# Attention to experts: rows and gate logits of a tile from one product of 144 columns, with the partial logits added on VectorE

## The chip, the core and the metric

The kernel runs on one core of a Trainium2 chip. The time is device microseconds of one execution, from the first to the last instruction of the core and the short start and stop around them. Lower is better. The engines are named as the profile names them: PE is TensorE (PEld its weight loads), DVE VectorE, ACT ScalarE, POOL GpSimd, SP SyncE, which here only issues DMAs.

## What is computed

Three layers follow one another, all in float32. The core of the reference:

```
scores = q @ k.T / sqrt(64);  ret = scores * gamma[h] ** (i - j)   (i >= j, else 0);  x = ret @ v
logits = x @ w_gate;  noisy = logits + log1p(exp(x @ w_noise)) * noise
the two largest of 8 experts per row, softmax over the two
x = sum over the two of weight * (relu(x @ w1[e]) @ w2[e])
out = (h * cos(h)) @ w_out   with h = x @ w_in
```

There are 4 sequences of 576 positions, 8 heads of 64, so 2304 rows of 512 values, 8 experts with 1024 hidden values, and a last layer with 2048. The change is in the first stage alone: attention, gate logits and the routing of rows to experts.

## The kernel before

The 2304 rows are 18 tiles of 128. Attention is computed as a recurrence: a tile's own part by scores (L1607), scaled by the decay table (`scale`, L1164, VectorE), times v (L1630), and a carried part from a state of 64 x 64 per head (L1622), which each tile updates with a decayed k (`decay_k`, L1180) times v (L1638) and `carry` (L1172, VectorE) rescales. Nine tiles hold two sequences; the fifth of nine (steps 4 and 13) is mixed, its scaling takes six operations instead of two, and the ninth (tiles 8 and 17) updates no state.

The engines run in steps. In step s TensorE computes the scores of tile s, both parts of the output of tile s-1, the state update with s-1, and for tile s-2 the gate logits and the rows. The output of a tile comes out transposed (512 values by 128 rows); ScalarE copies it to `xT` (L779). From xT TensorE computes the 16 gate and noise logits (L1658: four products that accumulate into one of two banks, where the logits of a group of 3 to 4 tiles stay until they are used) and transposes xT back into rows (L1663: four transposes into bank 5). A float32 product is two instructions in the trace, a transpose is one. ScalarE copies the rows out (L789, `x_sb`), and signals `x_done`, on which the next transposes wait.

The order on each engine is the order of the code. On ScalarE a step is: softplus of a group of tiles (L755 to L763, in steps 6, 10, 14 and 17, with two loads of function tables), xT of tile s-1, the row copy of tile s-2, and in steps 4, 5, 8, 9, 13 and 16 (`SPLIT_AT`) the high part of a chunk of expert weights (w_hi, L745). On VectorE it is: scaling of tile s, carry of tile s-1, decayed k of tile s, then second choice with running totals (steps 7, 11, 15, 18), ranks to places (`place_rows`, L1141 on, steps 8, 12, 16), first choice (`first_choice`, L1110 on, steps 6, 10, 14, 17), and the low part of the weight chunk (w_lo, L1075). TensorE counts ranks (`count`, L1578 to L1583) in steps 8, 12, 16 and 18. The next scores wait for the scaling of the tile before. GpSimd multiplies q by the decay (L701) and scatters rows to the experts' slots in DRAM.

Behind step 19 follow the experts. Their first unit starts with two blocks of rows that were scattered early (transposes L1592, copies L767 and L1266), then products L1722 (first weights) and L1734 (second weights), with relu L822 on ScalarE and the low part L1274 on VectorE.

Of the kernel before, what the change touches and what calls it, by code (L numbers as in the profile page):

```python
# [23 lines left out]
P = 128  # L24
B, H, S, D = 4, 8, 576, 64
DM = H * D
C = P
# [25 lines left out]
TB = TPB * C  # L53
SIZES = (3, 5, 5, 5)
# [95 lines left out]
def build(nc, qk, kv, noise, gates_w, weights, pairs, table, out):  # L150
# [7 lines left out]
    with ExitStack() as ctx:  # L158
# [35 lines left out]
        with ExitStack() as st:  # L194
# [8 lines left out]
            wg = keep("wg", [P, KD_TILES, 2 * E], F32, st)  # L203
            used = -(-ATTN_W // 8) * 8 + 3 * 2 * DM + 3 * 2 * DM + 2 * DM + 2 * DM + DM // 2 + 3 * 2 * DM + 2 * DM + KD_TILES * 2 * E
# [11 lines left out]
            hots = keep("hots", [C, 2, NT * E], F32, st)  # L216
            before_sum = grid("before_sum", (NT + 1) * E)
# [55 lines left out]
        chain, soft_chain, soft_done = sem("chain"), sem("soft_chain"), sem("soft_done")  # L273
        picked_done, counted, ranked, pos_done = sem("picked_done"), sem("counted"), sem("ranked"), sem("pos_done")
# [45 lines left out]
        def logit_bank(k):  # L320

            return ps[7 - k % 2]
# [358 lines left out]
        def _(pool):  # L681
            nc.gpsimd.memset(zeros_sb[:, :], 0.0).then_inc(rows_zero, 1)

            def scatter_rows(t, k):
                pool.wait_ge(pos_done, group_of(t) + 1)
                pool.wait_ge(x_done, t + 1)
# [21 lines left out]
            for t in range(LATE_FROM, NT):  # L708
                if t == LATE_FROM:
                    pool.wait_ge(out_done, NT - 1)  # L710
                elif t == LATE_FROM + 1:
                    pool.wait_ge(out_done, NT)
                elif t == LATE_FROM + 2:
                    pool.wait_ge(logit_done, NT)
# [26 lines left out]
        def _(act):  # L741
# [5 lines left out]
            def softplus(k):  # L747
                lo, hi = GROUPS[k], GROUPS[k + 1]
                n = hi - lo
                act.wait_ge(logit_done, hi)  # L750
                if k == 0:
                    act.wait_ge(q_mixed_in, 16)
                above(act, picked_done, k)
                z = logit_bank(k)[0:C, 0:n * 2 * E].rearrange("c (t e) -> c t e", e=2 * E)[:, :, E:2 * E]
# [16 lines left out]
            def step(s):  # L771
# [3 lines left out]
                if 0 <= t < NT:  # L775
                    act.wait_ge(out_done, t + 1)
                    above(act, logit_done, t - 1)
# [6 lines left out]
                t = s - 2  # L784
                if t == NT - 1:
# [283 lines left out]
        def _(dve):  # L1069
# [34 lines left out]
            def first_choice(k):  # L1104
                lo, hi, n = tiles_of(k)
                both = logit_bank(k)[0:C, 0:n * 2 * E].rearrange("c (t e) -> c t e", e=2 * E)
# [23 lines left out]
            def place_rows(k):  # L1130
                lo, hi, n = tiles_of(k)
                bank = logit_bank(k)
# [33 lines left out]

            def carry(t):
# [132 lines left out]
            for j in range(FRONT[0]):  # L1300
                x_low(0, j)
            place_rows(NG - 2)
# [266 lines left out]
        def _(pe):  # L1569
            ident = tab("ident")  # L1570

            def count(k):
                lo, hi = GROUPS[k], GROUPS[k + 1]
                n, bank = hi - lo, logit_bank(k)
                pe.wait_ge(picked_done, k + 1)
                if k == 0:
# [19 lines left out]
            def step(s):  # L1596
# [51 lines left out]
                if 0 <= t < NT:  # L1648
                    k_ = group_of(t)
# [61 lines left out]
            def first1(f, part_no):  # L1711
# [4 lines left out]
                if part_no == 0:  # L1716
                    pe.wait_ge(split_done, f + 1)
                above(pe, hs_done, i - 1)
# [231 lines left out]
```

## Time and profile before

| | us |
|---|---|
| median of 3 runs | 964.93 (964.05 to 965.29) |
| the profiled execution | 967.21 |
| its span (first to last instruction) | 965.4 |
| TensorE busy in the span | 949.5 (98%) |
| VectorE busy | 557.5 (58%) |
| ScalarE busy | 474.5 (49%) |
| attention stage, first scores to first expert product | 5.6 to 99.4 |

The granted clock of TensorE is at full speed in all 40 slices of the span. The views used are: the chain of the work that ended last; busy time of each engine in chosen stretches; and the timeline, where instructions of one kind that follow one another are one row with their count, the first number is the start in us from the span's start, the second the time from the first start to the last end, and brackets at the end give the idle time ahead and what ended it.

### The profile page before, as it was taken

The numbers are of one execution on the slowest core, as the hardware profiler recorded it, in microseconds if no ns is written. First come the engines' busy times: TensorE is split into PE (matmuls) and PEld (weight loads), VectorE is DVE, ScalarE is ACT, GpSimd is POOL, SyncE is SP. The second block draws the span as 40 slices with busy tenths as digits, with TensorE's granted clock in tenths as the row PEclk, the third lists the DMA queues.
The fourth block names the chain that finished last, engine by engine and source line by source line (L and its number), as shares of the span: only waits on it lengthen the run. The fifth ranks groups of instructions, "written<-read, shape, count | busy, mean of one in ns | idle before, by whom it ended". The sixth has DMA issues, their size and how long they took to land.

```text
span 965.4 us, 17039 instructions
## 1 busy us (share of the span) xinstructions
PE 949.5 (98%) x6144; PEld 846.1 (88%) x6144; DVE 557.5 (58%) x1118; ACT 474.5 (49%) x889; POOL 95.0 (10%) x93
## 2 busy tenths in 40 slices
PE   8999899999999999999999999999999999999998
PEld 7988788988989889889898889888888888888987
DVE  4789554455555545534332145567777777776665
ACT  1445434434434344333232156567666765766555
POOL 2266600000000000000000123001100100000000
PEclk9999999999999999999999999999999999999999
DMA  9988546598879897874317259877666755656561
GB/s 363 325 329 284 197 161 231 175 299 307 294 281 316 292 329 249 261 253 135 122 65 270 68 169 326 279 277 259 241 256 226 263 216 234 237 205 238 218 236 55
DMA packets 77406, 230.29 MB, mean 239 GB/s; under 512 B 6781, under 2 KB 31005, under 8 KB 69149
## 3 DMA queue, kind: packets, MB, share of 16 engines
q1 hardware_dynamic: 71581, 210.58, 61.7%
q0 software_dynamic: 5760, 18.88, 5.4%
q8 instruction: 37, 0.61, 0.2%
q14 instruction: 28, 0.23, 0.1%
HBM read 167.75 MB, written 61.69 MB: 238 GB/s over the span
## 4 chain that ended last, share of the span: by engine, by line
PE 82%; DVE 7%; ACT 6%; issue 3%; DMA 2%; POOL 0%; SPq 0%; DVEq 0%
PE ps L1704 18%; PE ps L1686 17%; PE ps L1879 14%; PE ps L1865 11%; PE ps L1734 3%; PE ps L1722 3%; PE ps L1805 3%; PE ps L1793 2%; PE ps L1630 2%; PE ps L1607 2%; PE ps L1622 2%; ACT angle L968 2%; PE ps L1658 2%; PE ps L1592 2%; ACT angle L966 1%
## 5 line engine op out<-in xcount | busy, mean ns | idle before, releaser
L1879 PE MATMUL ps<-w_sb,g_hi 128*128 128x512 f32 x576 | 180.4, 394 | 0.1
L1686 PE MATMUL ps<-xs,w_hi 128*128 (+1 forms) x784 | 177.7, 308 | 0.0
L1287 DVE TENSOR_TENSOR w_lo<-raw,w_hi 128x1024 fp32r<-128x1024 f32 x48 | 58.8, 1225 | 157.2 <-ACT w_hi L807 157.2
L1686 PEld LDWEIGHTS ps<-xs,w_hi 128*128 128x128 f32 x784 | 131.7, 188 | 1.2
L1865 PE MATMUL ps<-x_odd,w_sb 128*128 128x320 f32 x672 | 117.7, 310 | 2.1 <-DVE h_sb L1442 1.2
L1686 PE MATMUL ps<-xs,w_lo 128*128 (+1 forms) x392 | 119.1, 304 | 0.0
L1865 PEld LDWEIGHTS ps<-x_odd,w_sb 128*128 128x128 f32 x672 | 106.2, 188 | 14.5 <-DVE h_sb L1442 2.5
L807 ACT ACTIVATE w_hi<-raw 128x1024 fp32r<-128x1024 f32 x48 | 50.8, 1058 | 129.6 <-PE ps L1704 126.1
L1879 PE MATMUL ps<-w_sb,g_lo 128*128 128x512 f32 x288 | 112.5, 391 | 0.0
L1879 PEld LDWEIGHTS ps<-w_sb,g_hi 128*128 128x128 f32 x576 | 101.0, 188 | 9.8 <-issue 0.3
L1704 PE MATMUL ps<-w_hi,hs_lo 128*128 128x512 f32 (+1 forms) x245 | 97.0, 396 | 0.0
L1704 PE MATMUL ps<-w_lo,hs_hi 128*128 128x512 f32 (+1 forms) x245 | 96.3, 393 | 0.0
L727 POOL DMA_INDIRECT y<-y_slots,pos_i x36 | 35.4, 982 | 615.5 <-SPq L647 429.2
L1704 PE MATMUL ps<-w_hi,hs_hi 128*128 128x512 f32 (+1 forms) x245 | 95.4, 389 | 0.0
L801 ACT ACTIVATE hs_hi<-ps 128x308 fp32r<-128x308 f32 x98 | 41.6, 424 | 68.0 <-PE ps L1686 68.0
L974 ACT ACTIVATE g_hi<-angle 128x320 fp32r<-128x320 f32 (+1 forms) x112 | 53.7, 479 | 43.2 <-DVE angle L1457 38.0
L966 ACT ACTIVATE angle<-angle 128x320 f32<-128x320 f32 (+1 forms) x112 | 53.5, 478 | 42.9 <-DVE angle L1451 41.3
L1686 PEld LDWEIGHTS ps<-xs,w_lo 128*128 128x128 f32 x392 | 73.7, 188 | 0.9
L1462 DVE TENSOR_TENSOR g_lo<-angle,g_hi 128x320 fp32r<-128x320 f32 (+1 forms) x112 | 56.1, 501 | 30.8 <-ACT g_hi L974 20.8
L1457 DVE TENSOR_TENSOR angle<-h_sb,angle 128x320 f32<-128x320 f32 x96 | 47.2, 491 | 45.5 <-ACT angle L968 43.7
L960 ACT ACTIVATE turns<-h_sb 128x320 f32<-128x320 f32 x96 | 44.9, 468 | 44.7 <-DVE h_sb L1440 41.6
L968 ACT ACTIVATE angle<-angle,table_sb 128x320 f32<-128x320 f32 (+1 forms) x112 | 64.0, 571 | 3.6
(193 smaller groups left out, 1606.2 us busy)
## 6 DMA issues: line engine op xcount, KB each, us to landing
w_sb<-w_pairs SPq DMA_DIRECT2D x24, 1792.0 KB, 7.7
w_sb<-w_pairs SPq DMA_DIRECT2D x40, 1024.0 KB, 10.0
raw<-weights SPq DMA_DIRECT2D x64, 512.0 KB
w_pairs<-stage SPq DMA_DIRECT2D x24, 1024.0 KB, 7.1
qk<-qk SPq DMA_DIRECT2D x18, 512.0 KB
kv<-kv SPq DMA_DIRECT2D x18, 512.0 KB
y_slots<-zeros_sb SPq DMA_DIRECT2D x33, 256.0 KB
gath<-x_slots SPq DMA_DIRECT2D x32, 256.0 KB, 6.5
```

The lines of the kernel that those rows point to most:

```text
L807: nc.scalar.activation(w_hi[:, f * CHUNK:(f + 1) * CHUNK], raw[:, f % 2, :], ACT.Copy).then_inc(hi_done, 1)
L960: nc.scalar.activation(turns[c % 2][:, 0:n], h[:, 0:n], ACT.Copy, bias=ROUND).then_inc(turn_done, 1)
L966: nc.scalar.activation(a, a, ACT.Abs).then_inc(abs_done, 1)
L968: nc.scalar.activation(a, a, ACT.Sin, scale=-2.0 * np.pi, bias=tab("half_pi")).then_inc(sin_done, 1)
L974: nc.scalar.activation(g_part(g_hi, slot, q), angle[c % 4][:, 0:width(slot)], ACT.Copy).then_inc(g_hi_done, 1)
L1287: tt(w_lo[:, at], raw[:, f % 2, :], w_hi[:, at].bitcast(F32), ALU.subtract).then_inc(split_done, 1)
L1457: tt(angle[c % 4][:, 0:n], h_of(slot, q)[:, 0:n], angle[c % 4][:, 0:n], ALU.mult).then_inc(g_done, 1)
L1462: tt(g_part(g_lo, slot, q), angle[c % 4][:, 0:n], g_part(g_hi, slot, q).bitcast(F32), ALU.subtract).then_inc(g_split, 1)
L1686: last_one = nc.tensor.matmul(ps[5 + half][:, 0:HALF], w[:, at:at + P], xs[:, bass.ds(g % 2, 1), a, k, half * HALF:(half + 1) * HALF].rear ...
L1704: last_one = nc.tensor.matmul(ps[j][0:ROWS[j], :], a[:, f % 2, rows_of(j)], w[:, at:at + DM], start=f == 0 and i == 0, stop=f == FE - 1 an ...
L1865: last_one = nc.tensor.matmul(p_bank(i)[:, 0:n], w[:, hl, cols], x[:, a, m, k, :], start=k == 0 and j == 0, stop=k == 1 and j == 2)
L1879: last_one = nc.tensor.matmul(ps[j][:, :], a[:, slot % 2, part, j * C:(j + 1) * C], w2_sb[slot % 3][:, hl, part * DM:(part + 1) * DM], sta ...
```

## The change

The gate weights in SBUF get 144 columns for each of the four parts of a row instead of 16: the 16 columns of weights and the 128 columns of a unit matrix, in this order or the other by turns. One product of such a part with xT gives the transposed rows and a partial sum of the logits. Two parts share a bank (5 and 6): they are laid so that the 16 logit columns of both fall on the same columns and accumulate. So each bank holds 256 row values and half of the logits. VectorE adds the halves into SBUF (`sum_logits`, new, two operations of 128 x 16), in step s for tile s-3, behind the scaling. TensorE's product waits for both row copies and for the sum of the tile before, and all readers of the logits read SBUF. The wait of the first tile of a group for earlier ranks is gone; rank counts all use bank 7. The row copy is two instructions of 256 columns. The last tile keeps four logit products (bank 4) and four transposes (bank 3), and the second chunk of the first expert product waits for its row copy. The sums of tiles 16 and 17 are made behind the experts' first `x_low`. In the last step the row copy stands ahead of the last softplus.

```diff
@@ ACT, step @@
                 t = s - 2
+                if 0 <= t < NT:
+                    act.wait_ge(rows_ps_done, t + 1)
+                    for k in range(0, KD_TILES, 2):
+                        rows = row_bank(k)[0:C, 0:2 * GW].rearrange("c (k d) -> c k d", d=GW)[:, :, 0:P]
...
+                        nc.scalar.activation(x_sb[t][:, k * P:(k + 2) * P].rearrange("c (k d) -> c k d", d=P), rows,
+                                             ACT.Copy).then_inc(x_done, 1)
                 if t == NT - 1:
                     softplus(NG - 1)
-                if 0 <= t < NT:
-                    act.wait_ge(rows_ps_done, t + 1)
-                    nc.scalar.activation(x_sb[t][:, :], ps[5][0:C, :], ACT.Copy).then_inc(x_done, 1)
@@ DVE @@
+            def sum_logits(t):
+                if t == NT - 1:
+                    dve.wait_ge(rows_ps_done, NT)
+                else:
+                    dve.wait_ge(x_done, 2 * t + 2)
+                logits = both_sb[:, t * 2 * E:(t + 1) * 2 * E]
+                if t == NT - 1:
+                    nc.vector.tensor_copy(logits, LAST_LOGITS[0:C, 0:2 * E]).then_inc(logit_done, 1)
+                else:
+                    nc.vector.tensor_copy(logits, row_bank(0)[0:C, P:P + 2 * E]).then_inc(half_done, 1)
+                    dve.wait_ge(half_done, t + 1)
+                    tt(logits, row_bank(2)[0:C, P:P + 2 * E], logits, ALU.add).then_inc(logit_done, 1)
...
             for s in range(NT + 1):
                 if s < NT:
                     scale(s)
+                if 0 <= s - 3 < NT - 2:
+                    sum_logits(s - 3)
                 if 0 < s <= NT and (s - 1) % CB < CB - 1:
                     carry(s - 1)
...
                 x_low(0, j)
+            for t in range(NT - 2, NT):
+                sum_logits(t)
             place_rows(NG - 2)
@@ PE, step @@
-                    if t == GROUPS[k_]:
-                        above(pe, ranked, k_ - 1)
                     pe.wait_ge(xT_done, t + 1)
-                    at = (t - GROUPS[k_]) * 2 * E
-                    for k in range(KD_TILES):
-                        last_one = nc.tensor.matmul(logit_bank(k_)[0:C, at:at + 2 * E], xT[t % 2][:, k, :], wg[:, k, :],
-                                                    start=k == 0, stop=k == KD_TILES - 1)
-                    last_one.then_inc(logit_done, 1)
-                    above(pe, x_done, t)
+                    if t == NT - 1:
+                        pe.wait_ge(state_done, updates(t))
...
+                        return
+                    above(pe, x_done, 2 * t)
+                    above(pe, logit_done, t)
                     for k in range(KD_TILES):
-                        last_one = nc.tensor.transpose(ps[5][0:C, k * P:(k + 1) * P], xT[t % 2][:, k, :], ident)
+                        at = P * (k % 2)
+                        last_one = nc.tensor.matmul(row_bank(k)[0:C, at:at + GW], xT[t % 2][:, k, :], wg[:, k, :],
+                                                    start=k % 2 == 0, stop=True, skip_group_check=True)
                     last_one.then_inc(rows_ps_done, 1)
```

How the work stands on VectorE around step 5 before the change (line, operation, output<-inputs, shape, and the semaphores waited for): the low part of a weight chunk, the scaling of tile 5, carry, decayed k.

```order
L1172 TENSOR_TENSOR state<-ps,attn_table 128x256 [waits u_done]
L1180 TENSOR_TENSOR k_dec<-kv,attn_table 128x512 [waits u_done,kv_in1]
L1075 TENSOR_TENSOR w_lo<-raw,w_hi 128x1024 [waits hi_done]
L1164 TENSOR_TENSOR ret<-ps,attn_table 128x512 [waits scores_done] x2
L1172 TENSOR_TENSOR state<-ps,attn_table 128x256 [waits u_done]
L1180 TENSOR_TENSOR k_dec<-kv,attn_table 128x512 [waits u_done,kv_in2]
```

The same place in the changed kernel, whose line numbers differ (L1177 is the scaling, L1198 carry):

```order
L1198 TENSOR_TENSOR state<-ps,attn_table 128x256 [waits u_done]
L1206 TENSOR_TENSOR k_dec<-kv,attn_table 128x512 [waits u_done,kv_in1]
L1088 TENSOR_TENSOR w_lo<-raw,w_hi 128x1024 [waits hi_done]
L1177 TENSOR_TENSOR ret<-ps,attn_table 128x512 [waits scores_done] x2
L1189 COPY both_sb<-ps 128x16 [waits x_done]
L1191 TENSOR_TENSOR both_sb<-ps,both_sb 128x16 [waits half_done]
L1198 TENSOR_TENSOR state<-ps,attn_table 128x256 [waits u_done]
L1206 TENSOR_TENSOR k_dec<-kv,attn_table 128x512 [waits u_done,kv_in2]
```

Two short operations stand between the scaling and carry; nothing else moved. On TensorE, the end of a step before:

```order
L1638 MATMUL ps<-kv,k_dec 64x64 [waits k_dec_done]
L1638 MATMUL ps<-kv,k_dec 64x64 x7
L1658 MATMUL ps<-wg,xT 128x16 [waits xT_done]
L1658 MATMUL ps<-wg,xT 128x16 x3
L1663 MATMUL ps<-table_sb,xT 128x128 [waits x_done]
L1663 MATMUL ps<-table_sb,xT 128x128 x3
L1607 MATMUL ps<-qk 128x128 [waits ret_done,qk_in0]
```

And in the changed kernel:

```order
L1669 MATMUL ps<-kv,k_dec 64x64 [waits k_dec_done]
L1669 MATMUL ps<-kv,k_dec 64x64 x7
L1698 MATMUL ps<-wg,xT 128x144 [waits logit_done,x_done,xT_done]
L1698 MATMUL ps<-wg,xT 128x144 x3
L1638 MATMUL ps<-qk 128x128 [waits ret_done,mixed_done,qk_in2]
```

Eight products and transposes became four products, and the first of them waits for the sum (`logit_done`) and the row copies (`x_done`) of the tile before.

## Rows read from the trace of the kernel before

**Rows 1.** The chain of work that ended last, shares of the span by engine.

```profile
PE 82%; DVE 7%; ACT 6%; issue 3%; DMA 2%; POOL 0%; SPq 0%; DVEq 0%
```

**Rows 2.** Busy time in stretches: steps 5, 9 and 10 of attention.

```profile
core 0: us, PE busy (x) PEld busy (x) DVE busy (x) ACT busy (x) POOL busy (x), PEclk, DMA share, GB/s
...
27.10:32.16 5.06, 5.06 (x78) 4.53 (x78) 3.47 (x6) 2.14 (x3) 1.27 (x1) 1.00 1.00 347
...
47.85:52.47 4.62, 4.62 (x62) 3.99 (x62) 3.17 (x5) 2.14 (x3) 2.77 (x3) 1.00 0.71 280
52.47:56.65 4.18, 4.06 (x61) 3.66 (x61) 2.44 (x4) 4.07 (x7) 3.70 (x4) 1.00 0.95 329
```

**Rows 3.** The chain in step 5: start us, us, engine, output, line, instructions.

```profile
27.09 1.09 PE ps L1607 x16
28.18 1.02 PE ps L1622 x16
29.20 1.02 PE ps L1630 x16
30.22 0.46 PE ps L1638 x16
30.68 0.99 PE ps L1658 x8
31.68 0.48 PE ps L1663 x4
```

**Rows 4.** Timeline of steps 4 and 5 (start us, us, engine, line, operation).

```profile
26.45 0.64 PE L1663 MATMUL ps<-table_sb,xT 128*128 128x128 f32 x4
...
27.12 0.60 ACT L789 ACTIVATE x_sb<-ps 128x512 f32<-128x512 f32 x1 [1.34 <-PE ps L1663]
27.61 1.05 ACT L745 ACTIVATE w_hi<-raw 128x1024 fp32r<-128x1024 f32 x1
...
28.70 1.22 DVE L1075 TENSOR_TENSOR w_lo<-raw,w_hi 128x1024 fp32r<-128x1024 f32 x1 [1.58 <-ACT w_hi L745]
...
29.84 1.28 DVE L1164 TENSOR_TENSOR ret<-ps,attn_table 128x512 f32<-128x512 f32 x2
```

**Rows 5.** Timeline of ScalarE and VectorE: softplus, first choice, scaling, steps 6 and 7.

```profile
33.64 0.19 ACT L755 ACTIVATE soft_a<-ps 128x32 f32<-128x32 f32 x1
...
35.40 0.32 ACT L760 ACTIVATE soft_a<-soft_b,attn_table 128x32 f32<-128x32 f32 x1
...
37.15 0.58 ACT L779 ACTIVATE xT<-ps 128x512 f32<-128x512 f32 x1
...
37.20 0.18 DVE L1110 SCALAR_TENSOR_TENSOR t_c<-ps,soft_a 128x32 f32<-128x32 f32 x1
37.41 0.19 DVE L1111 TENSOR_TENSOR t_b<-t_c,noise_sb 128x32 f32<-128x32 f32 x1
...
38.75 0.19 DVE L1101 TENSOR_TENSOR hots<-t_b,code 128x32 f32<-128x32 f32 x1
38.98 1.29 DVE L1164 TENSOR_TENSOR ret<-ps,attn_table 128x512 f32<-128x512 f32 x2
```

**Rows 6.** Timeline of ScalarE: two copies of 256 columns out of PSUM.

```profile
102.53 0.65 ACT L822 ACTIVATE hs_hi<-ps 128x256 fp32r<-128x256 f32 x2
```

**Rows 7.** Timeline of step 4, the mixed tile: scores, scaling's first and last operation.

```profile
21.93 1.16 PE L1607 MATMUL ps<-qk 64*128 64x128 f32 x16
...
23.20 0.27 DVE L1160 MEMSET ret<- 64x256 f32 x1 [1.18 <-PE ps L1607]
...
25.34 0.69 DVE L1164 TENSOR_TENSOR ret<-ps,attn_table 64x512 f32<-64x512 f32 x1
```

**Rows 8.** Timeline of TensorE at the stage's end, steps 17 to 19.

```profile
91.84 1.06 PE L1658 MATMUL ps<-wg,xT 128*128 128x16 f32 x8
...
96.30 0.96 PE L1658 MATMUL ps<-wg,xT 128*128 128x16 f32 x8
...
97.58 0.30 PE L1578 MATMUL ps<-picked,attn_table 128*128 128x24 f32 x2
...
99.43 0.36 PE L1722 MATMUL ps<-xs,w_hi 128*128 128x256 f32 x1
```

More of the change, by code:

```diff
@@ L53 @@
 TB = TPB * C
+GW = P + 2 * E
 SIZES = (3, 5, 5, 5)
@@ L202, in build @@
             xT = [keep(f"xT{i}", [P, KD_TILES, C], F32, st) for i in range(2)]
-            wg = keep("wg", [P, KD_TILES, 2 * E], F32, st)
-            used = -(-ATTN_W // 8) * 8 + 3 * 2 * DM + 3 * 2 * DM + 2 * DM + 2 * DM + DM // 2 + 3 * 2 * DM + 2 * DM + KD_TILES * 2 * E
+            wg = keep("wg", [P, KD_TILES, GW], F32, st)
+            used = -(-ATTN_W // 8) * 8 + 3 * 2 * DM + 3 * 2 * DM + 2 * DM + 2 * DM + DM // 2 + 3 * 2 * DM + 2 * DM + KD_TILES * GW
             keep("below_rows", [P, 2 * RING * CHUNK + TPU * DM - used], F32, st)
@@ L216, in build @@
             hots = keep("hots", [C, 2, NT * E], F32, st)
+            both_sb = keep("both_sb", [C, NT * 2 * E], F32, st)
             before_sum = grid("before_sum", (NT + 1) * E)
@@ L318, in group_of, with row_bank, logits_of @@
             return next(k for k in range(NG) if GROUPS[k] <= t < GROUPS[k + 1])
-        def logit_bank(k):
-            return ps[7 - k % 2]
+        def row_bank(k):
+            return ps[5 + k // 2]
+        def logits_of(t, n):
+            return both_sb[:, t * 2 * E:(t + n) * 2 * E].rearrange("c (t e) -> c t e", e=2 * E)
+        COUNTS, LAST_LOGITS, LAST_ROWS = ps[7], ps[4], ps[3]
         def x2_bank(n):
@@ L784, in step @@
                 t = s - 2
+                if 0 <= t < NT:
[3 more added lines that the diff above has]
+                        if t == NT - 1:
+                            rows = LAST_ROWS[0:C, k * P:(k + 2) * P].rearrange("c (k d) -> c k d", d=P)
+                        nc.scalar.activation(x_sb[t][:, k * P:(k + 2) * P].rearrange("c (k d) -> c k d", d=P), rows,
+                                             ACT.Copy).then_inc(x_done, 1)
                 if t == NT - 1:
                     softplus(NG - 1)
-                if 0 <= t < NT:
-                    act.wait_ge(rows_ps_done, t + 1)
-                    nc.scalar.activation(x_sb[t][:, :], ps[5][0:C, :], ACT.Copy).then_inc(x_done, 1)
                 if s in SPLIT_AT:
@@ L1105, in first_choice @@
                 lo, hi, n = tiles_of(k)
-                both = logit_bank(k)[0:C, 0:n * 2 * E].rearrange("c (t e) -> c t e", e=2 * E)
+                both = logits_of(lo, n)
                 if k == 0:
@@ L1131, in place_rows @@
                 lo, hi, n = tiles_of(k)
-                bank = logit_bank(k)
+                bank = COUNTS
                 dve.wait_ge(counted, k + 1)
@@ L1573, in count @@
                 lo, hi = GROUPS[k], GROUPS[k + 1]
-                n, bank = hi - lo, logit_bank(k)
+                n, bank = hi - lo, COUNTS
                 pe.wait_ge(picked_done, k + 1)
+                above(pe, ranked, k)
                 if k == 0:
@@ L1652, in step @@
                         pe.wait_ge(wg_in, 16)
-                    if t == GROUPS[k_]:
-                        above(pe, ranked, k_ - 1)
                     pe.wait_ge(xT_done, t + 1)
-                    at = (t - GROUPS[k_]) * 2 * E
-                    for k in range(KD_TILES):
-                        last_one = nc.tensor.matmul(logit_bank(k_)[0:C, at:at + 2 * E], xT[t % 2][:, k, :], wg[:, k, :],
-                                                    start=k == 0, stop=k == KD_TILES - 1)
-                    last_one.then_inc(logit_done, 1)
-                    above(pe, x_done, t)
-                    for k in range(KD_TILES):
-                        last_one = nc.tensor.transpose(ps[5][0:C, k * P:(k + 1) * P], xT[t % 2][:, k, :], ident)
+                    if t == NT - 1:
+                        pe.wait_ge(state_done, updates(t))
+                        for k in range(KD_TILES):
+                            at = P * (1 - k % 2)
+                            nc.tensor.matmul(LAST_LOGITS[0:C, 0:2 * E], xT[t % 2][:, k, :], wg[:, k, at:at + 2 * E],
+                                             start=k == 0, stop=k == KD_TILES - 1)
+                        for k in range(KD_TILES):
+                            last_one = nc.tensor.transpose(LAST_ROWS[0:C, k * P:(k + 1) * P], xT[t % 2][:, k, :], ident)
+                        last_one.then_inc(rows_ps_done, 1)
+                        return
+                    above(pe, x_done, 2 * t)
+                    above(pe, logit_done, t)
+                    for k in range(KD_TILES):
+                        at = P * (k % 2)
+                        last_one = nc.tensor.matmul(row_bank(k)[0:C, at:at + GW], xT[t % 2][:, k, :], wg[:, k, :],
+                                                    start=k % 2 == 0, stop=True, skip_group_check=True)
                     last_one.then_inc(rows_ps_done, 1)
@@ L1717, in first1 @@
                     pe.wait_ge(split_done, f + 1)
+                    if f == 1:
+                        pe.wait_ge(x_done, 2 * NT)
                 above(pe, hs_done, i - 1)
@@ L1932 @@
     rows = moe2_w_out.reshape(FP, 2, P, DM).transpose(0, 2, 1, 3).reshape(FP, P, 2 * DM)
-    gates = np.concatenate([moe_w_gate, moe_w_noise], axis=1).reshape(KD_TILES, P, 2 * E).transpose(1, 0, 2)
+    gates = np.concatenate([moe_w_gate, moe_w_noise], axis=1).reshape(KD_TILES, P, 2 * E)
+    unit = np.eye(P, dtype=np.float32)
+    gates = np.stack([np.concatenate([unit, g] if k % 2 == 0 else [g, unit], axis=1) for k, g in enumerate(gates)], axis=1)
     arrays = {
```

9 lines of the change are left out of this document (4 added, 5 removed).

## The prediction

> **What bounds the kernel now.** I read the chain of work that ended last first: 82% of its span is TensorE [rows 1]. Then the busy time by stretch, over steps of the attention stage: TensorE is busy for all of a step's 5.06 us and for all of the 4.62 us of step 9 [rows 2]. So the 18 tiles cost what TensorE's own instructions cost, and the stage is worth shortening. The chain of one step, step 5 [rows 3], gives the parts: scores 1.09 us, carried part 1.02, own part 1.02, state update 0.46, the four logit products 0.99, the four row transposes 0.48. That is 5.06 us, and the logits are reached 3.59 us after the scores begin (30.68 against 27.09).
>
> Then the timeline of the same step, for the slack of the others [rows 4]. VectorE scales the scores of step 5 only from 29.84, though they are ready at about 28.2: ahead of the scaling stands w_lo (28.70), which waits for w_hi (27.61), which stands on ScalarE behind the copy of the rows (27.12), which waits for the transposes of the step before, ended at 27.09. The scaling ends at 31.12. Today nothing needs it before the next scores at 32.16, so a lateness of one microsecond costs nothing. This is the cover that the change uses up.
>
> **What it removes.** Four transposes (0.48 us) and four 16-column products (0.99) become four products of 144 columns, eight instructions instead of twelve. A 16-column piece takes 0.99/8 = 124 ns, so it is paced by loading 128 weight columns and not by its columns. How long 144 columns take no row shows. Below: 0.99 us, if the load still paces them. Above: pairs of half-array products take 0.46/8 = 58 ns at 64 columns and 1.02/8 = 128 ns at 128 [rows 3], 1.09 ns for each column more, which makes 145 ns at 144 and 1.16 us for eight. I take the middle, 1.07: 0.40 us less a tile, and 17 tiles give 6.8 us. The last tile keeps its 1.47.
>
> The Trainium skill speaks against this trade: Perfetto Trace Analysis, section Transposes, says that a logical transpose should be a transpose and not a standard matmul, since transposes skip the arithmetic. By that rule the unit columns would cost a pass of their own and the product would save nothing, 1.47 us. The rows speak against the rule here, since the weight load is paid by the logits anyway; it is a rival below.
>
> **What it adds.** On VectorE, right behind each scaling, two [128 x 16] operations that sum the logits of the tile three back. The product of step s now waits for that sum, since both banks are used again. The nearest operations take 0.18 us, follow one another in 0.21 where the second waits for the first (37.20, 37.41) and overlap the next by 0.08 where it doesn't (28.70 + 1.22 against 29.84) [rows 4, 5]. So a sum ends 0.30 us behind the scaling, TensorE restarts 0.10 later, and VectorE loses 0.31 a step; bounds 0.20 (nothing waited for) and 0.42 (both in full). On the dependence between the two: the Trainium skill, VectorE: DVE Perf Modes, section The DRAIN you can't avoid, says that an operation starts only when the pipe is empty, semaphore or not. That would make it 0.42 and the forecast 1.3 us later; w_lo and the scaling overlap by 0.08 us here, so the trace doesn't agree.
>
> The row copy in two halves costs 0.65 against 0.60 us [rows 4, 6]. The weights of the gates grow from 32 to 288 KB; at the rate of the first stretches that is under a microsecond of a queue whose next users have more slack, and I cost it at nothing; without the cover it is 0.7 us.
>
> **What becomes late.** TensorE's own step would be 5.07 - 0.40 = 4.67 us. Three kinds of steps can't be that short.
>
> Steps 5, 6, 9, 10, 14 and 17, whose scaling stands behind w_lo. From the end of the transposes to the end of the scaling it is 31.12 - 27.09 = 4.03 us; the second copy adds 0.05, the sum and the restart 0.40, the product and its end 1.17. This closes a circle (product, row copy, w_hi, w_lo, scaling, sum, product) of 5.65 us. Four of these steps take 5.07 now: 4 x 0.58 = 2.3. Steps 9 and 10 lack a part of TensorE's work and take 4.62 and 4.18 [rows 2], so they lose 1.03 and 1.47. Together 4.8 us.
>
> Steps 7, 11 and 15, behind a first choice. Softplus now waits for the sum behind the scaling: 2.08 us of ScalarE (33.64 to 35.72), 1.78 of first choice (37.20 to 38.98), 1.29 of scaling [rows 5], 0.30 of sum and 0.1 of handovers make 5.55 from product to product. 3 x 0.48 = 1.4 us.
>
> Steps 4 and 13, where the tile has two sequences: its scaling goes from 23.20 to 26.03, which is 4.10 us after the scores began at 21.93 [rows 7]. With 0.40 the product starts at 4.50 instead of 3.59: 0.9 less the 0.40 saved is 0.5. In step 13 VectorE comes from placing ranks and is later still, I take 0.8. Together 1.3 us.
>
> Steps 2, 3, 8, 12 and 16 wait for nothing and keep the gain, 5 x 0.40 = 2.0 us.
>
> The stage up to step 18: 4.8 + 1.4 + 1.3 - 2.0 = 5.5 us later. Then step 18: the sum of tile 15 waits for its row copy, and that copy stands on ScalarE behind softplus, table loads and xT. From the sum of tile 14: 3.51 us (33.64 to 37.15), 0.49, 0.65 and 0.4 make about 5.1 between the two products, now 4.46 (91.84 to 96.30) [rows 5, 8]: 0.6. Behind that sum stands the second choice with its totals, 2.24 us, and the rank count waits for it: 2.3 us after the product, now 1.28 (96.30 to 97.58): 1.0. The last tile (logits 0.99, transposes 0.48) and the first expert product behind it (now 99.43) follow as now, and I see nothing that gives time back: the experts' first half starts with data that was long loaded, and its late rows are scattered on a count of TensorE's own products. Sum: 5.5 + 0.6 + 1.0 = 7.1, say 7.0 us. The profiled execution takes 967.21 us (span 965.4 and 1.8 around it) and would take 974.2; from the median 964.93 it is 971.9.
>
> Bounds: product 0.99 and sum 0.20 take 1.3 and 1.3 us off (16 steps, 12 waits), product 1.16 and sum 0.42 add 1.4 and 1.3: 969.3 to 974.6.
>
> **Rivals.** (a) The waits don't come and the gain stays: 964.93 - 6.8 = 958.1, faster. One mechanism: VectorE reaches the sum before TensorE reaches the product. For this the scaling would have to end 0.4 us before product time, 3.59 us into a step; in step 5 it ends at 4.03, in step 4 at 4.10. The point from which it decides is 0.9 us of lateness; what speaks for it are only the five steps in which VectorE is in time. (b) The circles hold loosely, waits of half the size: +1 to +4 us, about 967.4. For it: steps are coupled, and a late TensorE lets VectorE catch up. Against it: each circle contains the product itself, so lateness doesn't cure it. (c) The unit columns cost a pass, product 1.47, which lengthens the twelve late steps by 0.40 each: +4.8, 976.7. (d) Waits and gain cancel, within 0.2%: seven waits instead of twelve.
>
> **Chances.** Forecast (969.3 to 974.6) 0.72, (a) 0.10, (b) 0.08, (c) 0.05, (d) 0.05. 0.2% is 1.9 us, about what a measurement of this kernel can tell from no change: faster 0.10, same 0.05, slower 0.85. The range reaches to (b) and (c), 966.5 to 976.8, and leaves (a) and most of (d) out.
>
> **What would show it.** After: eight 144-column pieces in 1.0 to 1.16 us; TensorE idle ahead of the product, released by the sum, twelve times with 0.9 to 2 us, some 13 us in all; steps of 5.65 us where w_lo stands ahead and of 4.67 in steps 3, 8 and 16; VectorE's scaling and sum back to back; first expert product at about 106.5 instead of 99.43, and the same length behind it. It is wrong if TensorE's idle time ahead of the product is under 5 us, if the product takes over 1.3 us, or if the experts' part changes by more than a microsecond.

## The result and the profile after

The changed kernel takes 980.29 us (median of 4 runs, 978.89 to 982.29) against 964.71 beside it: ratio 1.0153, 95% interval 1.0137 to 1.0168. It is slower, and by more than forecast: 971.9 with a range up to 976.8. The profiled execution has a span of 977.6 us (979.43 in all) against 965.4. The traces so show 12.2 us of difference, where the medians show 15.6; the profiled execution of the kernel before lies 2.5 us above its median, that of the changed one 0.9 below. What follows is about the 12.2; the other 3.4 no trace shows.

What TensorE waited for in the changed kernel, in all three layers (engine, output and line, releaser: us in total, times, longest). L1698 is the product of 144 columns, L1191 the sum, L1623 the transposes of late rows, L1818 the transposes in the last layer.

```profile
PE ps L1698 <- DVE both_sb L1191: 12.5, 12, 2.0
PE ps L1623 <- DMA gath<-x_slots: 3.7, 3, 3.0
PE ps L1818 <- DVE y L1411: 2.1, 1, 2.1
```

Twelve waits, 12.5 us, from 0.7 to 2.0 us each. The prediction said twelve, 0.9 to 2 us, some 13 in all, and they stand in the twelve steps that it named. The chain that ended last, cut to step 5 (start us, us, engine, output, line, instructions), answers to [rows 3], which was TensorE alone from start to end:

```profile
26.24 1.23 PE ps L1698 x8
27.47 0.02 issue
27.50 0.03 ACT x_sb L799
27.52 0.25 issue
27.77 0.38 ACT x_sb L799
28.15 0.96 ACT w_hi L754
29.11 0.02 issue
29.13 1.23 DVE w_lo L1088
30.36 1.20 DVE ret L1177 x2
31.55 0.09 DVE both_sb L1189
31.65 0.02 issue
31.67 0.18 DVE both_sb L1191
31.86 0.14 issue
31.99 1.23 PE ps L1698 x8
```

This is the circle, link by link: product, row copy, high part, low part, scaling, sum, product again, 31.99 - 26.24 = 5.75 us. The same stretch in the timeline (brackets: idle time ahead, and what ended it), which answers to [rows 4]:

```profile
28.04 1.06 ACT L754 ACTIVATE w_hi<-raw 128x1024 fp32r<-128x1024 f32 x1
...
29.13 1.23 DVE L1088 TENSOR_TENSOR w_lo<-raw,w_hi 128x1024 fp32r<-128x1024 f32 x1 [2.11 <-ACT w_hi L754]
...
30.27 1.28 DVE L1177 TENSOR_TENSOR ret<-ps,attn_table 128x512 f32<-128x512 f32 x2
...
31.99 1.22 PE L1698 MATMUL ps<-wg,xT 128*128 128x144 f32 x8 [0.93 <-DVE both_sb L1191]
```

VectorE's 2.11 us of idle time ahead of w_lo are the heart of it. VectorE is idle for want of ScalarE's high part, and the scaling and the sum that TensorE needs stand behind.

The lengths of the steps, from the first scores of one to those of the next:

| step | 2 | 3 | 4 | 5 | 6 | 7 | 8 | 9 | 10 | 11 | 12 | 13 | 14 | 15 | 16 |
|---|---|---|---|---|---|---|---|---|---|---|---|---|---|---|---|
| before | 5.07 | 5.08 | 5.08 | 5.08 | 5.08 | 5.08 | 5.53 | 4.62 | 4.25 | 5.08 | 5.75 | 5.07 | 5.08 | 5.08 | 5.53 |
| after | 4.77 | 4.78 | 5.81 | 5.75 | 5.75 | 5.64 | 5.22 | 5.75 | 5.75 | 5.56 | 5.45 | 6.04 | 5.75 | 5.56 | 5.23 |

The end of the stage on TensorE, which answers to [rows 8]. L1653 is the carried part, L1609 the rank count, L1688 and L1691 logits and transposes of the last tile, L1760 the first expert product, L1772 the first one with second weights:

```profile
99.44 1.22 PE L1698 MATMUL ps<-wg,xT 128*128 128x144 f32 x8 [0.93 <-DVE both_sb L1191]
100.59 1.09 PE L1653 MATMUL ps<-q_dec,state 64*64 64x128 f32 x16
...
104.61 1.22 PE L1698 MATMUL ps<-wg,xT 128*128 128x144 f32 x8 [0.88 <-DVE both_sb L1191]
106.51 0.40 PE L1609 MATMUL ps<-picked,attn_table 128*128 128x24 f32 x2 [0.68 <-DVE before_sum L1137]
...
106.97 1.54 PE L1688 MATMUL ps<-wg,xT 128*128 128x16 f32 x8
108.35 1.09 PE L1691 MATMUL ps<-table_sb,xT 128*128 128x128 f32 x4
109.10 0.56 PE L1760 MATMUL ps<-xs,w_hi 128*128 128x256 f32 x1
...
114.29 0.40 PE L1772 MATMUL ps<-w_hi,hs_hi 128*128 128x512 f32 x1
```

The last tile's logits, whose instructions are those of before, take 1.38 us from start to start (106.97 to 108.35) instead of 1.08 in the same place before (97.94 to 99.02), and its transposes 0.75 (to 109.10) instead of 0.41 (to 99.43). The reason stands in the busy time by stretch (stretch, PE busy, PEld, DVE, ACT, POOL, then the granted clock):

```profile
104.61:106.90 2.29, 1.61 (x12) 1.40 (x12) 2.01 (x10) 1.49 (x4) 0.60 (x1) 1.00 0.55 213
106.90:114.20 7.30, 7.30 (x39) 7.30 (x39) 4.17 (x20) 2.88 (x7) 3.53 (x4) 0.53 0.24 94
114.20:118.00 3.80, 3.80 (x24) 3.41 (x24) 2.62 (x14) 1.07 (x3) 0.75 (x2) 1.00 0.25 96
```

For 7.3 us TensorE runs at a granted clock of 0.53, about the lower of its two levels (1.2 instead of 2.4 GHz), while it is busy all the time. In the eight us before 106.5 it had waited 0.93, 0.88 and 0.68 us. In the kernel before the clock is full in this place.

So the difference grows along the trace: +7.3 us at the carried part of tile 17 (100.59 against 93.32), +8.3 at the last wide product (104.61 against 96.30), +8.9 at the rank count, +9.7 at the first expert product, +10.9 at the first second-weights product (114.29 against 103.42), +11.3 at the experts' second part, +11.1 at the start of the last layer, +12.2 at the end, the last step of it behind the one wait of 2.1 us at L1818 above.

### The profile page after: what moved, and what is told of

Read it like the earlier page. It is cut to its first block, busy times and chain, and to the rows that moved or that the text cites. A ratio compares the mean times of both kernels' runs of the same rounds, so it can differ in the third digit from the quotient of the medians.

```text
span 977.6 us, 16976 instructions
## 1 busy us (share of the span) xinstructions
PE 947.7 (97%) x6076; PEld 844.3 (86%) x6076; DVE 559.9 (57%) x1153; ACT 476.2 (49%) x907; POOL 95.2 (10%) x93
## 4 chain that ended last, share of the span: by engine, by line
PE 72%; DVE 10%; ACT 8%; issue 5%; DMA 3%; POOL 1%; SPq 0%; DVEq 0%; POOLq 0%
PE ps L1740 17%; PE ps L1722 17%; PE ps L1917 13%; PE ps L1903 11%; PE ps L1831 2%; PE ps L1843 2%; PE ps L1772 2%; ACT angle L981 2%; PE ps L1623 2%; PE ps L1760 2%; DVE angle L1487 2%; ACT angle L979 2%; DVE ret L1177 1%; PE ps L1698 1%; DVE angle L1481 1%
```

## The experiments

All ratios are to the kernel before, run on the same chip in turns. Line numbers in rows of an experiment are its own.

**1. The wait without the product.** The kernel before, its products and transposes as they were, with two dummy operations on VectorE where the sum would stand, and TensorE's logit product waiting for them:

```diff
                 if s < NT:
                     scale(s)
+                if 0 <= s - 3 < NT - 2:
+                    extra(s - 3)        # copy and add, 128 x 16, on its own memory
@@ PE @@
+                    if t < NT - 1:
+                        above(pe, extra_done, t)
```

> The kernel before, with the wait alone: two small VectorE operations on spare data (128 x 16, the second waits for the first) behind each scaling from step 3 on, and TensorE's logit products of step s wait for them as the wide product does in the changed kernel. Products, transposes, banks and row copies stay as before. Theory (the wait behind the scaling is the whole cost): TensorE waits some 11 us in twelve steps, the first expert product starts at 111 to 113 us, time 978 to 986. Rival (the wide product, its banks and the halved row copies are what costs): within 2 us of the kernel before, 964.7.

Measured: 985.24 us, ratio 1.0197 (1.0182 to 1.0212). Its first expert product starts at 119.74 us, 20.3 later than before and some 7 later than expected. Steps 13, 14 and 16 take 6.81, 6.47 and 6.47 us (scores at 82.34, 89.15, 95.62, then 100.69 and 107.16) where they took 5.07, 5.08 and 5.53; step 16 does not even wait in the changed kernel. The clock is full in these steps, so this is the wait itself.

It is not so in the whole stage. The rows show TensorE's waits for the two operations, then the stretch from the scores of step 2 to the first expert product, with the same instructions but for one, here and in the kernel before:

```profile
PE ps L1670 <- DVE extra_sb L1172: 10.4, 8, 2.2
12.16:119.74 107.58, 97.19 (x1267) 87.06 (x1267) 76.35 (x212) 40.37 (x67) 41.80 (x37) 0.90 0.76 267
11.78:99.43 87.65, 87.50 (x1266) 78.63 (x1267) 68.91 (x177) 39.55 (x66) 43.72 (x37) 1.00 0.91 326
```

Of the 19.9 us that the stretch is longer, some 10.2 are waiting and 9.7 are the same work at a lower granted clock: 0.90 in the mean, 0.50 in 60 to 66 us, behind a wait of 2.2 us. So the added wait, with the clock that falls when it comes, is enough to lose more than the change loses. The waits alone are not: they are 10.4 us, where the changed kernel has 12.5.

**2. The same work, waited for by nobody.** The same two operations, without the two lines on PE.

> The kernel before with two more operations of 128 x 16 on VectorE behind each scaling, the second waiting for the first, as the changed kernel has them, but on memory of their own, and no other engine waits for them. The same two operations with TensorE's logit product waiting for them gave 985.2 us against 965.8. Theory (the wait costs, not the work): 0.3 us of VectorE a step move the scaling of steps 5 and others a little, but the next scores had a microsecond of slack; 965.5 to 968. Rival (VectorE is so full that its load alone sets the steps, the wait only shows it): 16 x 0.31 us come through in most of the late steps, 970 or more.

Measured: 968.60 against 968.40, ratio 1.0009 (1.0000 to 1.0018). Its first expert product is 2.0 us late (101.42), and at the end of the span 1.3 of that are left against the trace of before (966.7 and 965.4). So of the 2% of experiment 1 about 1.9 come with the wait, half of it as waiting and half as a lower clock: VectorE is 58% busy in the span and has time for the work; it does not have it at the moment at which TensorE asks.

This trace holds something else: the clock falls behind the rank count here too, though TensorE had waited 0.27 us in the ten before 101.2. A stretch just behind the first expert product:

```profile
102.00:103.00 1.00, 1.00 (x6) 1.00 (x6) 0.29 (x2) 0.98 (x2) 0.88 (x1) 0.50 0.21 82
```

So a fall of the clock needs no long wait just ahead of it.

**3. The sum ahead of the scaling.** The changed kernel, with the sum of the tile three back ahead of the scaling of this step:

```diff
             for s in range(NT + 1):
+                if 0 <= s - 3 < NT - 2:
+                    sum_logits(s - 3)
                 if s < NT:
                     scale(s)
-                if 0 <= s - 3 < NT - 2:
-                    sum_logits(s - 3)
```

> The changed kernel, with one edit: VectorE sums the logits of tile s-3 ahead of the scaling of tile s instead of behind it. Nothing else moves. Theory (the circles through the scaling make the changed kernel slow): the row copies of tile s-3 are done by then, so VectorE doesn't wait, TensorE's idle time ahead of the wide product falls from about 13 us in all to under 4, steps come down from 5.75 to 4.8 us, and the first expert product starts at about 97 us against 109.1 in the changed kernel and 99.4 in the one before. With few waits the clock stays at full level. Time 961 to 963.5 us. Rival (the wide product of 1.17 us and VectorE's added work cost what was lost, wherever the sum stands): it stays above 975.

Measured: 967.77, ratio 1.0029 (1.0013 to 1.0044). Of the 1.53% over the kernel before 1.24 are gone, some 12 us, with two instructions moved by one place. The waits for the sum fall from 12.5 us to

```profile
PE ps L1698 <- DVE both_sb L1191: 2.2, 4, 0.9
```

and steps 5, 6, 9 and 10 from 5.75 us each to 4.78, 4.78, 4.61 and 4.71. The mixed tiles come down to 4.77 and 5.03 (steps 4 and 13), two of the three steps behind a first choice to 5.02 and 4.78 (7 and 15); step 11 stays at 5.80, and no run tells why. But the expected 961 to 963.5 did not come. The first expert product starts at 98.53, 0.9 us ahead of the kernel before and not the 2.4 of the expectation: step 18 stayed long. And what was gained there was spent behind it: TensorE reaches the late rows earlier and waits 2.2 us for their DMA at 123.68, the clock is 0.50 in 126 to 130, and the last layer has a wait of 2.1 us at L1818.

**4. The high part first.** The changed kernel with the other link of the circle opened: on ScalarE the high part of the weight chunk ahead of the row copy, the sum where the change has it.

```diff
                 t = s - 2
+                if s in SPLIT_AT:
+                    split_high(SPLIT_AT[s], w_hi, SPLIT_AT[s] * CHUNK)
                 if 0 <= t < NT:
                     act.wait_ge(rows_ps_done, t + 1)
...
-                if s in SPLIT_AT:
-                    split_high(SPLIT_AT[s], w_hi, SPLIT_AT[s] * CHUNK)
```

> The changed kernel, with one edit on ScalarE: in the six steps that split a weight chunk, w_hi stands ahead of the row copy of tile s-2 instead of behind it. Theory (in steps 5, 6, 9, 10, 14 and 17 the circle product, row copy, w_hi, w_lo, scaling, sum, product of 5.75 us sets the time): the circle is cut, those six steps lose 0.6 to 1.9 us each, about 7 us together, while the steps behind a first choice and the mixed ones keep their waits. First expert product at about 102, time 971 to 974. Rival (VectorE is simply out of time in these steps, in whatever order): no change from 980.3.

Measured: 974.43, ratio 1.0097 (1.0083 to 1.0112), just above the expected 971 to 974; the first expert product starts at 102.49. Steps 5, 6, 9 and 10 take 4.78, 4.78, 4.46 and 4.71 us; the mixed tiles (5.80 and 6.05) and step 11 (5.80) are as late as in the changed kernel, since high parts have nothing to do with them. The clock is 0.74 in 98 to 104 us. The waits for the sum are 4.7 us in six.

```profile
PE ps L1698 <- DVE both_sb L1191: 4.7, 6, 1.2
```

Experiments 3 and 4 open the same circle at two different links and both times the 5.75-us steps are gone. That is what shows the circle, and rules out the product and a general lack of time on an engine.

**5. The clock.** The changed kernel, with seven products of zeros in step 18, whose results nobody reads: four ahead of the last wide product, three ahead of the rank count, where TensorE had waited anyway.

```diff
                     above(pe, logit_done, t)
+                    if t == NT - 2:
+                        fill(4)
...
                 if t == NT - 2:
+                    fill(3)
                     count(NG - 2)
```

> The changed kernel, with dummy products of zeros into the spare bank 7 in step 18: four ahead of the last wide product and three ahead of the rank count, where TensorE waited 0.9 and 0.7 us. They should fit into the waits. Theory (the granted clock fell to 0.53 from 106.9 to 114.2 because TensorE had waited just before, and 3.4 us of the loss are this clock): the clock stays at full level there, the first unit's products take 119 ns instead of 213, and the time is 2.5 to 3.5 us less, about 977. Rival (the fall has nothing to do with these two waits, but with the ones before them or with something else): the clock falls all the same, 980.

Measured: 975.92, ratio 1.0114 (1.0099 to 1.0128), 4.4 us less than the changed kernel by the medians, 3.8 by the ratios. Products that compute nothing make the kernel faster. The mean granted clock of its four executions is 0.996 to 0.998, that of the changed kernel's four 0.991 to 0.995. Its stretch that answers to 106.90 to 114.20 above, with clock 1.00:

```profile
106.90:114.20 7.30, 6.71 (x50) 6.24 (x51) 5.08 (x22) 3.19 (x8) 3.84 (x4) 1.00 0.29 108
```

The rank count is even 0.3 us later than without (106.84), but the first expert product comes at 108.59 instead of 109.10 and the first second-weights product at 112.31 instead of 114.29.

By the traces the kernel is 4.9 us faster (spans 972.7 and 977.6). 2.0 of them are there at the second-weights product, 1.1 more at the experts' second part (138.66 against 141.73), behind a shorter wait for the late rows (2.2 against 3.0 us). Another 2.0 come in the last layer, where this trace lacks the wait of 2.1 us; nothing shows that the fill did that.

**6. Both moves.** Experiments 3 and 4 in one kernel.

> The changed kernel with both moves at once: the sum of the tile three back stands on VectorE ahead of the scaling, and the high part of a weight chunk stands on ScalarE ahead of the row copy. Each alone took part of the circle apart: with the sum first 2.2 us of waiting on it were left, with the high part first 4.7. Theory (the loss is the order of the queues, and two handovers make it): the waits on the sum in steps 5 to 17 go to under 1 us in all, the carried product of tile 17 starts at about 88.6 us of the span (before 93.3, sum first alone about 91.2), the first expert product at about 97 (before 99.43, sum first alone 98.53). Behind it the stall for the late rows stays, since their scatters are paced by the experts' own products and TensorE only reaches it earlier. So the time is 964 to 967 us by the stall and the halved clock behind it, 963 if the gain of the stage is kept. Rival (the stage is held by something else, VectorE's own load): the first expert product stays at 98.5 and the time at 967.8.

Measured: 967.01 against 968.40, ratio 0.9987 (0.9976 to 0.9998). The stage is now clearly shorter than before (steps 5, 6, 9, 10 at 4.78, 4.78, 4.32, 3.82), but the first expert product comes at 98.16, not at 97. TensorE still waits in step 18, and the clock falls once more behind it (0.80 in 98 to 104):

```profile
93.91 1.22 PE L1698 MATMUL ps<-wg,xT 128*128 128x144 f32 x8 [0.51 <-DVE both_sb L1191]
95.86 0.40 PE L1609 MATMUL ps<-picked,attn_table 128*128 128x24 f32 x2 [0.73 <-issue]
```

**7. Both moves, and a fill for the late rows.** Seven products of zeros ahead of the transposes of the first late rows.

```diff
+            fill(7)
             for j in range(FRONT[0], TPU):
                 transpose_x(0, j)
```

> The kernel with both moves, and seven more float32 products of 128 columns of zeros (14 instructions, some 1.85 us by the 0.26 us that one took in the filled step 18) into the bank of the rank counts, ahead of the transposes of the first late block of rows, where TensorE waited 2.2 us with the sum first. Their results are read by nobody. Theory (a halved clock follows a wait of TensorE, and the products only use time in which it waits anyway): the granted clock stays full behind the stall, where the kernel with the sum first had 0.69 in 122 to 126 us and 0.50 in 126 to 130, which cost it some 3 us; the time is 2 to 3.5 us below the kernel with both moves alone and ends at 961 to 963.5, below the kernel before. Rival (the halved clock is a matter of the moment or of the DMA traffic, not of the wait): the clock falls all the same and the time is that of the kernel without the fill, or up to 1 us above it.

Measured: 967.19, ratio 0.9994 (0.9981 to 1.0007), the same as without. The clock is full from 104 us on, where experiment 6 had 0.71 in 122 to 126, and the second part starts at 128.37 instead of 129.11. That does not bear out the theory: the fill runs from 123.70, and experiment 6 lost its clock before that, behind a wait of 2.5 us at 119.54 that the profile calls "issue" and that is 1.0 us here. The expected 2 to 3.5 us were a misreading: in experiment 6 the long stall was no longer at the late rows, so there was nothing to fill there. And this execution had one wait of 2.77 us for the sum, in the attention stage at 60.05, where experiment 6 had 0.95; it is not explained.

**8. The table load out of step 18's chain.** With both moves, ScalarE still does in step 17: softplus, a load of the next function table (1.28 us), the output copy of tile 16, the row copy of tile 15. The load moves behind the two copies.

```diff
-                if k < NG - 1:
+                if k < NG - 2:
                     nc.scalar.activation(sin_ready[:, :], tab("half_pi"), ACT.Exp)
@@ behind the row copy @@
+                if s == NT - 1:
+                    nc.scalar.activation(sin_ready[:, :], tab("half_pi"), ACT.Exp)
```

> The kernel with the sum and the high part first, and in step 17 the load of the exponential's table (1.28 us of ScalarE) stands behind the output copy of tile 16 and the row copy of tile 15 instead of ahead of them. With both moves alone these copies started at 92.16 and 92.63 us though their data was there from 88.3 and 90.0, the sum of tile 15 waited for them until 93.38, TensorE's last wide product waited 0.51 us for that sum and the rank count behind it 0.73 us, and the granted clock was 0.88 in 94 to 98 and 0.80 in 98 to 104. Theory (step 18 is a chain softplus, table, copies, sum, second choice, count): the wide product no longer waits, the count comes 0.5 to 0.9 us earlier, the first expert product at 97.0 to 97.6 instead of 98.16; 1 us off the time, ratio to before 0.9965 to 0.998. Rival (the first choice on VectorE, which ends at 92.4, holds step 18 just as well, or the time is lost again at the late rows): the first expert product within 0.3 us of 98.16, ratio 0.9985 or more.

Measured: 965.44 against 967.75, ratio 0.9980 (0.9966 to 0.9994). The wide product no longer waits, the rank count waits 0.55, and the clock stays full in 94 to 104 us (it is 0.58 in 118 to 122, behind a wait of 2.4 us). The first expert product starts at 96.19, earlier than expected:

```profile
92.74 1.15 PE L1700 MATMUL ps<-wg,xT 128*128 128x144 f32 x8
94.44 0.40 PE L1611 MATMUL ps<-picked,attn_table 128*128 128x24 f32 x2 [0.55 <-issue]
...
96.19 0.36 PE L1762 MATMUL ps<-xs,w_hi 128*128 128x256 f32 x1
```

**9. And a fill ahead of the count.** The same with `fill(3)` ahead of `count(NG - 2)`.

> The same kernel, and three products of zeros (0.83 us for three in the filled step 18) between the last wide product and the rank count, where TensorE waited 0.73 us for the second choice. Theory (it is the wait just ahead that halves the clock of the experts' first products): the granted clock is full in 96 to 104, where both moves alone had 0.80 to 0.88 (some 1.3 us lost there), the experts' first pieces follow each other in 119 ns from the start, and the second part (columns of 360) starts 1 to 1.5 us earlier than with the table load alone; ratio to before 0.995 to 0.997. Rival (what is gained ahead of the late rows is lost waiting for them): the clock is full, and the time is that of the kernel with the table load alone.

Measured: 965.10 against 967.75, ratio 0.9975 (0.9963 to 0.9988): the best kernel of the study, faster than the kernel before by 0.25%; it can't be told from experiment 8. The time is where the rival put it. The clock is full in 94 to 104:

```profile
94.00:104.00 10.00, 9.31 (x70) 8.56 (x69) 7.34 (x35) 5.56 (x15) 5.95 (x7) 1.00 0.53 210
```

but it was full without the fill too, so the fill had nothing to save here. The experts' second part starts at 125.04 us, 2.3 ahead of experiment 8 and not the expected 1 to 1.5; this trace lacks that one's wait of 2.4 us and the lower clock behind it, and nothing shows that the fill is the reason. That is 5.4 us ahead of the kernel before, and at the end of the span 1.8 are left. Most of it goes at one row:

```profile
PE ps L1826 <- DVE y L1413: 3.6, 1, 3.6
```

In the last layer TensorE waits 3.6 us for rows that are gathered from DRAM. ScalarE, which is ahead of VectorE on the same rows, had waited for the DMA itself:

```profile
578.73 0.72 ACT L899 ACTIVATE y<-y,gate 128x512 f32<-128x512 f32 x1 [3.88 <-DMA y<-y_slots,pos_i]
```

Behind TensorE's wait the granted clock is 0.81 in 581.2 to 590 us. The kernel before and experiments 1, 2 and 5 have no such wait, experiments 3, 4 and 8 and the changed kernel do (2.1, 2.0, 3.3 and 2.1 us), experiments 6 and 7 a shorter one (0.9 and 0.6). In that stretch the gathers share the DMA engines with loads of 1 MB of weights. Which order of the two makes the wait was not tried and stays open.

## Why the prediction was right in kind and wrong in size

**The direction and the mechanism held.** The three kinds of late steps are the ones that were named, and each is late by about what its circle asks for. Experiments 3 and 4 show the circle through w_lo; for the other two kinds it is the size, and that moving the sum shortens them but for step 11, that speaks for the circle. By kind, forecast and measured against the kernel before (the circle steps are 5, 6, 9, 10, 14 and 17, the last by 94.84 to 100.59 against 88.24 to 93.32; step 10 of before is 4.25 us from scores to scores, not the 4.18 of the prediction's window):

| steps | forecast | measured |
|---|---|---|
| circle through w_lo (6) | +4.8 | +5.3 |
| behind a first choice: 7, 11, 15 | +1.4 | +1.5 |
| mixed tiles: 4, 13 | +1.3 | +1.7 |
| no wait: 2, 3, 8, 12, 16 | -2.0 | -1.5 |
| start, steps 0 and 1 | 0 | +0.3 |
| up to the carried part of tile 17 | +5.5 | +7.3 |

**The product was mis-sized.** "I take the middle, 1.07." It took the upper bound. The one that waits for nothing in step 18 of experiment 8 takes 1.15 in the timeline; from the start of a waited product to the next instruction it is 31.99 to 33.14, also 1.15. In steps without a wait it is 1.18 (20.40 to 21.58), and the saving was 0.30 (5.07 to 4.77) instead of 0.40. The line drawn through two other shapes, 58 ns at 64 columns and 128 at 128 [rows 3], gave 1.16; the middle between it and "the load still paces them" had no row on its side. At 0.08 to 0.10 in each of 16 steps that is 1.3 to 1.6 of the 1.8 us missing in the stage; the rest is in the mixed tiles and the first two steps. In these the wait for the first queries and keys (L1638) is 0.9 us where it was 0.8; it is 1.1 in experiment 1 too, whose gate weights are those of before, so it does not speak for the larger weights. The circle came out 5.75 against 5.65 for it.

The rule of the Trainium skill weighed in the prediction (Perfetto Trace Analysis, section Transposes) was not borne out here: the unit columns cost no pass of their own, 1.15 to 1.18 us for the wide product against 1.47 for products and transposes apart.

**The sum was sized right.** 0.30 behind the scaling: the scaling's end is at 31.55 and the sum's at 31.85 (31.67 + 0.18). The 0.10 to TensorE's restart is 0.14. What the prediction says there against the Trainium skill (VectorE: DVE Perf Modes, section The DRAIN you can't avoid) leaves out half of it: the same section says that an operation which is not held back starts earlier, so the overlap of 0.08 us here is no evidence against it.

**Step 18 held, but the sum counted 0.4 twice.** The forecast's 0.6 is from product to product, and there it measured 0.7 (99.44 to 104.61, 5.17 against 4.46). But the 5.5 us ahead of it end where the carried part of tile 17 begins, so the product's saving in step 17 was taken off once more. From the carried part on, the prediction's own terms give 5.1 - 1.07 = 4.0 against 2.98 now, +1.0, and +1.0 was measured (4.02). So its own terms sum to 7.5 and not 7.1. From the last wide product to the rank count it was +0.6 (forecast 1.0): the count came 1.90 us behind the product and not 2.3. The two errors cancel, which is luck.

**"I see nothing that gives time back", and nothing that takes any: this step failed.** Behind the rank count the forecast was a difference that stays at 7.1, and behind the first expert product "the same length"; the cost of a lower clock stood in the sum at nothing, without a reason. The difference grew from 8.9 to 12.2, 2.5 of it behind the first expert product, where the prediction had called more than a microsecond a sign of being wrong. Of these 3.3 us, 1.9 are the clock between rank count and second weights (0.7 up to the first expert product, 1.2 up to the first product with second weights). Experiment 5 shows it: with TensorE kept busy in its waits, the same stretch runs at full clock, and the second weights start 2.0 us earlier. The section on the profile before says "at full speed in all 40 slices", and the prediction took the clock for granted. A 9 in that row of the page only means 90% or more. The trace of before had a warning in it that I did not use: behind its one long stall of TensorE in the experts' first part, the granted clock is 0.77 between 118.5 and 126 us; a slice of the page is 24 us wide and hides that. Another 1.1 us come in the last layer with its wait of 2.1. The last 0.3 is spread.

**The rivals.** (a) and (d) did not come. (b) was wrong in saying that lateness lets VectorE catch up; the waits were all there. (c) was wrong in mechanism, but its 976.7 was nearer to the time than the forecast, for a reason that it did not contain. The range ended 3.5 us below the result. Against the forecast of 7.0 us the trace is 5.2 over: 1.8 in the stage, nothing in step 18 by cancelling errors, 3.3 behind it, and rounding. The medians are another 3.4 over, and no trace says where.

## What to carry to other kernels

When an instruction is put behind another on an in-order engine and a third engine waits for it, walk the whole way round: from the waiting product back to the product before. If the way closes, its length is the length of the step, no matter how idle each engine is. The remedy is the order in the queue; here it cost nothing (0.3 us of work ahead of the scaling instead of behind it: some 12 us).

Price a TensorE that starts to wait often at more than its waits: experiment 1 had 10.4 us of waits and lost another 9.7 to a lower clock. Look at the granted clock of short stretches, not of the page's slices, behind each place where it waits already.

A gain in a stage that is followed by a chain with its own pace (here scatters, gathers, weight loads) has to be followed to the end of the span: 5.4 us of lead at the experts' second part were worth 1.8 at the end.

## What was not expected of the hardware

The granted clock fell to 0.53 after three waits of 0.7 to 0.9 us within eight, not after a long one, and stayed there for 7.3 us of unbroken work. With waits of 0.51 and 0.73 us in the same place (experiment 6) it was 0.80 in 98 to 104 us, with 0.28 and 0.68 (experiment 3) or one of 0.55 (experiment 8) it stayed full, and with hardly any (0.27 in ten us, experiment 2) it fell. The earlier waits of the changed kernel, one of up to 2.0 us in each late step, did not lower it: step 5, in which TensorE was busy 4.82 of 5.75 us, has a clock of 1.00, and so have 12 to 99 us as a whole, with 75.83 us busy of 87. Nor did the one wait of 2.77 us in experiment 7 (1.00 in 60 to 70 us). In experiment 1 waits of 1.3 us did: behind the one that ended at 27.33 the clock is 0.68 in 28.8 to 33.9. So filling the waits kept the clock up in experiment 5, but the length of the last wait does not say when it falls. What of the activity counts, the runs don't tell.

Eight pieces of 144 columns took 1.15 to 1.18 us and eight of 16 columns 0.99, so 128 columns more cost 20 to 24 ns a piece; a transpose of 128 columns by itself costs 0.48 / 4 = 120 ns. Nine times the columns for a sixth more time is a good price; it was only paid at the wrong moment.

Between two 128 x 16 operations of VectorE of which the second waits for the first lie 0.02 us (31.65 to 31.67), and the second starts 0.20 after the first (31.47 and 31.67 in the timeline).
